# Keys and queries of tiles 0 to 4 in one transfer of 128 rows each, in place of two of 64 rows

## What is computed

```python
# q, k, v: batch 2, heads 8, 768 positions, 64 per head; n_global 8, n_local 96
scores = (1 / sqrt(64)) * q @ k.T
keep   = (key < n_global) | (0 <= query - key < n_local)
scores = where(keep, scores - slope(head) * distance, -1e9)
x = softmax(scores) @ v                      # then [1536, 512]

h  = x @ w_in                                # 512 -> 1024
s  = h * softmax(h)
x  = ((s - mean(s)) / sqrt(var(s) + 1e-6) * g_ln) @ w_out

h  = x @ w2_in                               # 512 -> 2048
out = (h * sigmoid(h)) @ w2_out
```

## Time and profile before

| | |
|---|---|
| time, median of 3 runs | 489.7 us (489.23 to 490.84) |
| the profiled execution's own time | 491.4 us |
| its span, first to last instruction | 489.4 us |
| TensorE matmul busy | 480.2 us, 98% of the span |
| VectorE, ScalarE, GpSimd busy | 302.5, 273.2, 220.5 us |
| moved by DMA | 44.38 MB, mean 91 GB/s |
| chain that ended last | PE 94%, SP's queue 3%, DMA 2% |

### The profile page before, as it was taken

How to read it: one execution, slowest core, us unless ns; L and a number is a source line. 1 busy time by engine, 2 the same in 40 slices (tenths; PEclk the granted TensorE clock), 3 DMA queues, 4 the chain that set the end, 5 groups by cost and what they waited for, 6 DMA issues and landing times.

```text
span 489.4 us, 8015 instructions
## 1 busy us (share of the span) xinstructions
PE 480.2 (98%) x2757; PEld 412.7 (84%) x2757; DVE 302.5 (62%) x729; ACT 273.2 (56%) x607; POOL 220.5 (45%) x288
## 2 busy tenths in 40 slices
PE   8889999999999999999999999999999999999997
PEld 5557888888888888888899988988999988988995
DVE  6778755585675676666575658665565546545542
ACT  5688646576576576755854454454454454344422
POOL 6427307678678679331624431444125431444200
PEclk9999999999999999999999999999999999999999
DMA  7994103533532642402222202221016202220003
GB/s 204 252 255 119 39 3 100 159 82 80 160 100 62 160 109 54 126 0 88 87 86 88 86 5 82 86 87 50 38 64 238 86 7 80 87 86 2 0 1 129
DMA packets 20522, 44.38 MB, mean 91 GB/s; under 512 B 2624, under 2 KB 8704, under 8 KB 20480
## 3 DMA queue, kind: packets, MB, share of 16 engines
q1 hardware_dynamic: 20160, 43.47, 30.4%
q10 hardware_dynamic: 320, 0.37, 0.2%
HBM read 40.69 MB, written 3.15 MB: 90 GB/s over the span
## 4 chain that ended last, share of the span: by engine, by line
PE 94%; SPq 3%; DMA 2%; issue 0%; DVE 0%; ACT 0%
PE hidden_ps L1193 24%; PE x_ps L1028 14%; PE hidden_ps L979 11%; PE score_ps L1216 9%; PE x_t_ps L1216 5%; PE x_ps L1216 5%; PE probs_t_ps L1216 5%; PE turn_ps L1216 5%; PE x_t_ps L966 4%; PE probs_t_ps L930 4%; PE turn_ps L1009 2%; DMA staged_q_raw<-q_t 2%; PE hidden_ps L996 2%; PE score_ps L898 1%; PE score_ps L899 1%; PE score_ps L919 1%
## 5 line engine op out<-in xcount | busy, mean ns | idle before, releaser
L874 POOL TENSOR_TENSOR wo_lo<-w_raw,wo_hi 128x512 fp32r<-128x512 f32 x32 | 41.4, 1316 | 145.5 <-ACT wo_hi L1463 145.5
L1475 ACT ACTIVATE act_hi<-mix_c 128x384 fp32r<-128x384 f32 x64 | 33.7, 526 | 96.5 <-DVE mix_c L1854 96.1
L732 POOL TENSOR_SCALAR probs<-probs,exp_inv 128x232 f32<-128x232 f32 x72 | 34.7, 499 | 49.3 <-DVE exp_inv L1625 48.1
L1296 ACT ACTIVATE probs<-logits,low_logit 128x232 f32<-128x232 f32 x96 | 45.5, 477 | 2.2 <-DVE low_logit L1612 1.9
L1854 DVE TENSOR_TENSOR mix_u<-hidden_ps,mix_p 128x384 f32<-128x384 f32 x16 | 8.9, 558 | 57.0 <-PE hidden_ps L1193 57.0
L1028 PE MATMUL x_ps<-w_out_hi,u_hi 128*128 128x512 f32 x96 | 40.6, 423 | 0.0
L1859 DVE TENSOR_TENSOR act_lo<-mix_c,act_hi 128x384 fp32r<-128x384 f32 x64 | 36.1, 567 | 6.3 <-ACT mix_c L1476 5.5
L1028 PE MATMUL x_ps<-w_out_hi,u_lo 128*128 128x512 f32 x96 | 37.9, 395 | 0.0
L1028 PE MATMUL x_ps<-w_out_lo,u_hi 128*128 128x512 f32 x96 | 37.5, 391 | 0.0
L979 PE MATMUL hidden_ps<-w_in_hi,x_hi 128*128 128x512 f32 x80 | 32.9, 411 | 0.0
L1612 DVE CUSTOM_DVE_ANT_0 logits<-score_ps,bias 128x232 f32<-128x232 f32 x88 | 30.6, 395 | 3.4 <-issue 3.4
(11 more groups left out here) (215 smaller groups left out, 1444.8 us busy)
## 6 DMA issues: line engine op xcount, KB each, us to landing
w_raw<-w SPq DMA_DIRECT2D x16, 1024.0 KB, 4.9
v_sb<-v_win SPq DMA_DIRECT2D x22, 224.0 KB
late_k_raw<-k_t SPq DMA_DIRECT2D x16, 232.0 KB, 4.2
k_raw<-k_t SPq DMA_DIRECT2D x14, 232.0 KB, 3.7
out<-out_sb SPq DMA_DIRECT2D x12, 256.0 KB, 2.1
w_in_raw<-w_in SPq DMA_DIRECT2D x4, 512.0 KB, 9.7
w_out_raw<-w_out SPq DMA_DIRECT2D x4, 512.0 KB, 14.3
late_q_raw<-q_t SPq DMA_DIRECT2D x16, 128.0 KB, 3.9
```

The costliest lines, as they stand in the source:

```text
L732: last = nc.gpsimd.tensor_scalar(probs[p][:, e, :], probs[p][:, e, :], exp_inv[:, p, e:e + 1], 0.0, ALU.mult, ALU.add)
L874: nc.gpsimd.tensor_tensor(wo_lo[j % 2][:, c, :], w2_raw[j % 2][:, c, BANK:2 * BANK], wo_hi[j % 2][:, c, :].bitcast(F32), ALU.subtract).the ...
L1296: last = nc.scalar.activation(probs[p][:, e, :], logits[b][:, e, :], ACT.Exp, scale=-1.0, bias=low_logit[:, b, e:e + 1], accum_out=exp_sum ...
L1475: nc.scalar.activation(act_hi[c][:, :], mix_c[c][:, :], ACT.Silu)
```

## The change

Tile 0's halves and its two issuers for each tensor go: SP issues the keys of both units as one transfer, ACT the queries of both as one. `load_early` does the same for tiles 1 to 4, both from SP. The semaphore of each tile now reaches 32 with two transfers where it reached 64 with four, and `first_half_loaded` is gone, so that both halves of tile 0's scores wait for the whole tile. One filler more runs ahead of them. The order of everything else stays.

```diff
-    def load_first(eng, unit):
-        rows = slice(unit * DH, unit * DH + DH)
-        for half, loaded in enumerate((first_half_loaded, early_loaded[0])):
-            keys = slice(half * 2 * KEYS, (half + 1) * 2 * KEYS)
-            queries = slice(half * 2 * P, (half + 1) * 2 * P)
-            eng.dma_start(staged_k_raw[rows, keys], k_v[0, unit][:, keys]).then_inc(loaded, 16)
-            eng.dma_start(staged_q_raw[rows, queries], q_v[0, unit][:, queries]).then_inc(loaded, 16)
...
                 keys, queries = raw_of(t, 0)
-                for unit in range(2):
-                    sp.dma_start(keys[unit * DH:unit * DH + DH, :], k_v[t, unit]).then_inc(early_loaded[t], 16)
-                for unit in range(2):
-                    sp.dma_start(queries[unit * DH:unit * DH + DH, :], q_v[t, unit]).then_inc(early_loaded[t], 16)
+                sp.dma_start(keys[:, :], k_v[t]).then_inc(early_loaded[t], 16)
+                sp.dma_start(queries[:, :], q_v[t]).then_inc(early_loaded[t], 16)
...
             sp.dma_start(spans_i[:, :], spans).then_inc(spans_loaded, 16)
-            load_first(sp, 1)
+            sp.dma_start(staged_k_raw[:, :], k_v[0]).then_inc(early_loaded[0], 16)
             load_early(1)
...
-                if t == 0 and half == 0:
-                    pe.wait_ge(first_half_loaded, 64)
-                elif t == 0 or half == 0:
-                    pe.wait_ge(early_loaded[t], 64)
+                if half == 0:
+                    pe.wait_ge(early_loaded[t], 32)
...
-            keep_warm(7)
+            keep_warm(8)
...
-            load_first(act, 0)
+            act.dma_start(staged_q_raw[:, :], q_v[0]).then_inc(early_loaded[0], 16)
```

More of the change, by code:

```diff
@@ L274, in attention_then_two_blocks @@
     zeros_made = sem("zeros_made")
-    first_half_loaded = sem("first_half_loaded")
     dist_made = sem("dist_made")
```

## The result

The kernel with the change takes 544.66 us (median of 6 runs, 544.21 to 545.25) against 490.03 (6 runs, 488.70 to 490.94): a ratio of 1.1111, 95% interval 1.1094 to 1.1129. It is **54.6 us slower**; forecast were 549 us, in a range of 529 to 590. The profiled execution has a span of 542.9 us, 53.5 longer than before.

The account below looks back on a forecast made before the run. TensorE's in-order queue bounds the kernel, without slack after tile 4's first scores at 46.32 us. On two engines tile 4 lands at 2.0 + 97.0 + 5.5 = 104.5: +58.2, restart +1.0, on 489.7 gives 549 us, range 529 to 590.

Parts of the forecast that it names:

- Two engines per merged transfer: Loads of tiles 0 to 4: source's outermost count 2 puts each merged transfer on two DMA engines; 0.83 within 529 to 590.
- Rival A: Merged loads: the destination's 128 rows govern, sixteen engines, not slower, likely -0.4 us, 489.3 us; chance 0.12.
- Tile 4's landing decides: TensorE waits for tile 4's queries, landing at 104.5 us, instead of starting its scores at 46.3: +58.2 us.
- +1 for +1: TensorE's queue after tile 4's first scores: any delay beyond 46.32 us delays the end one for one.
- The pace of keys and queries: Each of the two engines moves keys, queries and weights at 21.7 kB/us, bounds 15.6 and 25.8.
- rival C: Two engines at full pace, 25.8 kB/us each: 531 us; counted inside the forecast's range, no separate chance.
- Weights and values: Ahead of tile 4's queries: 262 kB of weights per engine at 21.7 kB/us, values 98 kB at 17.9, 5.5 us.
- The restart: TensorE after a long wait: 7 x 0.15 = 1.0 us extra, bounds 0 and 3.
- Rival B: Two engines that also run dry or hold up SP's issuing queue: over 590 us; chance 0.05.
- a sign that missed: DMA row: 1 or 2 tenths for most of the first 100 us, at 40 to 60 GB/s.
- All else costs nothing: Softmax of tiles 0 to 3, weight splits and the eighth filler (about 0.4 us) lie in the waits, costing nothing.
- Issues on ACT: ACT's queue: one issue less frees nothing, since its tables wait for VectorE until 5.56 us.

Follow-up runs that it names:

- the kernel with 128 outermost: Changed kernel, but tiles 0 to 4 read from a host copy with the 128 rows one behind the other, two dimensions: 488.80 us, ratio 0.9960.
- The run by parity: Kernel before, but tiles 1 to 4's two 64-row transfers, read from a host copy, fill even and odd partitions: 488.34 us, ratio 0.9964.
- the filled wait: Changed kernel with 26 more fillers of 512 columns ahead of the transposes before tile 4's first scores: 542.15 us.
- the pair of 488.80 and 488.79: Changed kernel reading tiles 0 to 4 from a host copy, 128 rows in two dimensions, with eight fillers (488.80 us) and with seven (488.79 us).

## Why the prediction was right, and where its terms were off

- **Two engines per merged transfer: right**, shown by 19,902 packets, the 2 end packets of q10, a share of 0.13, and by the row of kernels in which only the source's outermost count was changed. Rival A (0.12) is refuted: the source's count has a say. Its gain was also priced too low: it said 0.4 us, and at most tile 2's wait of 1.14. On sixteen engines the kernel with 128 outermost is 1.8 below the kernel before next to it (488.80 and 490.58), with tile 4's scores 2.3 us earlier; TensorE no longer waits for tile 1 (0.90 before) either. The run by parity shows where that comes from: spread over all partitions, transfers move faster.
- **Tile 4's landing decides: right for the change** (it waits there 5.89 us), as was +1 for +1 behind it: 50.7 us of later scores and 2.9 of restart make 53.6, the span grew by 53.5. With four or eight engines it did not hold.
- **The pace of keys and queries: too low.** For "I take 21.7" the runs measured 25.5 kB/us, rival C's 25.8 in practice. Five tiles take 1,843 / 25.5 = 72 us, not 85.
- **Weights and values: too cheap.** They had 262 / 21.7 + 5.5 = 17.6 us. Of the 97.1 us, 2 for the start and 72 for the tiles leave 23. In their stretches all sixteen engines run and each makes 238 / (0.84 x 16) = 17.7 kB/us (25 to 35 us); at that pace they need 20. Of the 3 left over, about 2 lie at the start: the two engines don't move 53 GB/s from 2.0 us on, but 25 from 2 to 4, 39 from 4 to 6 and 46 from 6 to 8. The two errors, -13 and +5, partly cancel: luck of about 5 us, which leaves tile 4 at 97.1 against 104.5. Without it the sum would have been some 5 us farther off, and the time still inside the range.
- **The restart: too cheap.** Two fillers' rows gave 1.0; it was 2.9, and the filled wait showed it to be the clock. The upper bound of 3 rested on 3 us of work at half speed, for which no row stood; the work at 0.51 lasted 6.48.
- **Rival B: half of it came, without its price.** SP stood 12.95 us on one issue. But the queues that ran dry were the fourteen that did not matter; two engines' share, 0.13, was there in the stretches of pure keys and queries (10 to 15 us, 45 to 50 us). The standing does show in a sign that missed: the DMA row was to stand at 1 or 2 tenths, 40 to 60 GB/s, for most of the first 100 us, and does so in three of its first seven slices. The sum let values and weights run beside the tiles; issued late, they come in bursts between them.
- **All else costs nothing: right.** The shift of the scores and the restart make the whole growth of the span, so the softmax and the splits moved no end; the eighth filler is worth nothing by the pair of 488.80 and 488.79.
- **Issues on ACT: misread.** The prediction has one less; it is three (q10 falls from 320 packets, four transfers of 80, to 130, one). Its conclusion holds: ACT's first work starts at 5.56 us in both.

## What to carry to other kernels

Before two transfers are merged into one, write down both access patterns: if one side's outermost dimension became small (a unit, a head, a batch), the transfer runs on that many DMA engines, however many partitions it fills (2, 4 and 8 were tried here; counts that are no power of two were not). Lay the rows out on the host so that they are one dimension, or choose the halves so that each spreads over all partitions; the packet count of the page, less the data rows, tells how many engines took part. And a wait of some microseconds ahead of TensorE costs more than its length, unless fillers keep its clock up.

## What the runs showed that was not expected

- A single DMA engine moves 25.5 kB/us when only two work, as much as each of sixteen does in the best microsecond of the 1 MB weight transfers (25.8); in the saturated stretch of the kernel before each makes 15.2.
- Transfers of 64 rows into one half of the partitions, queued one after the other, run at 251 to 260 GB/s in all, the same rows dealt by parity at 300.
- With 8 as the outermost count the stretch from 10 to 15 us moves 190 GB/s at a share of 1.04, 11.4 kB/us for each of sixteen. It stays open what holds it there.
- After an idle time of 5.9 us TensorE worked at a granted clock of 0.51 for 6.5 us, which cost 2.9; with the wait filled it worked at 1.00.
